# Attention with q and k laid out head dimension first, the output steps last in each tile's slot and the third part of the tiles in two banks

## The reference

```python
q_pool = q.reshape(B, H, S // 2, 2, D).mean(axis=3)          # B 2, H 8, S 1152, D 64
scores = scale * np.matmul(q_pool, k.transpose(0, 1, 3, 2))
attn = np.exp(scores - np.max(scores, axis=-1, keepdims=True))
attn = attn / (np.sum(attn, axis=-1, keepdims=True) + 1e-09)
attn_out = np.matmul(attn, v)                                # 16 heads of [576, 64]
x = attn_out.transpose(0, 2, 1, 3).reshape(B * S // 2, H * D)
x = (sigmoid(x @ w_gate) * (x @ w_val)) @ w_out              # 512 -> 1536 -> 512
# then 8 experts: out += P[:, e] * (relu(x @ w1[e]) @ w2[e]), P from a router
```

## Time and profile before

| | |
|---|---|
| median of 3 runs | 1294.13 us (1292.77 to 1295.09) |
| the profiled execution, its own time | 1293.19 us |
| its span in the profile | 1291.4 us |
| PE busy over the span | 1258.4 us (97%) |
| DVE, ACT, POOL busy over the span | 58%, 46%, 44% |
| attention: first exponential to last tile's exponential | 10.84 us to 292.33 us |
| granted TensorE clock in every slice | full |

### The profile page before, as it was taken

One profiled execution on the slowest core, in us unless ns is written; L12 is line 12 of the kernel. 1 busy time (PEld: TensorE's weight loads), 2 busy tenths in 40 slices (PEclk: granted clock), 3 DMA queues, 4 the chain that ended last, 5 costly groups with the idle time before them and its releaser, 6 DMA issues.

```text
span 1291.4 us, 20081 instructions
## 1 busy us (share of the span) xinstructions
PE 1258.4 (97%) x7716; PEld 1159.5 (90%) x7716; DVE 755.3 (58%) x1660; ACT 592.4 (46%) x1265; POOL 568.7 (44%) x336
## 2 busy tenths in 40 slices
PE   7999999989999999999999999999999999999999
PEld 6888888889999989999999899999998999999997
DVE  6888888885222313667656556556556465466443
ACT  6888888883333324444334334234333234234221
POOL 6466766680122247545325335335235245245211
PEclk9999999999999999999999999999999999999999
DMA  4334343211111043122222123123122122122112
GB/s 135 74 56 65 72 68 59 52 29 58 49 49 32 25 119 94 43 72 66 66 66 80 52 66 94 38 67 97 49 69 80 49 83 65 50 82 75 43 47 90
DMA packets 104090, 84.84 MB, mean 66 GB/s; under 512 B 14016, under 2 KB 80576, under 8 KB 104000
## 3 DMA queue, kind: packets, MB, share of 16 engines
q1 hardware_dynamic: 103856, 83.33, 24.3%
q10 hardware_dynamic: 144, 0.29, 0.1%
HBM read 79.15 MB, written 2.40 MB: 63 GB/s over the span
## 4 chain that ended last, share of the span: by engine, by line
PE 91%; DVE 4%; ACT 2%; issue 1%; POOL 1%; DMA 0%; SPq 0%; POOLq 0%; DVEq 0%; ACTq 0%
PE bank L957 11%; PE bank L959 11%; PE bank L958 11%; PE bank L1111 10%; PE bank L1112 10%; PE bank L1113 10%; PE bank L817 6%; PE bank L796 4%; PE bank L935 4%; PE bank L934 4%; PE bank L936 4%; PE bank L830 2%; PE bank L831 2%; PE bank L789 2%; DVE part_min L1441 2%
## 5 line engine op out<-in xcount | busy, mean ns | idle before, releaser
L1561 DVE TENSOR_TENSOR c<-bank,c 128x256 f32<-128x256 f32 (+1 forms) x448 | 197.2, 456 | 284.2 <-PE bank L959 273.7
L739 POOL TENSOR_TENSOR w_lo<-w_raw,w_hi 128x1024 fp32r<-128x1024 f32 x64 | 153.9, 2404 | 301.1 <-ACT w_hi L1128 301.1
L1112 PE MATMUL bank<-w_lo,h_hi 128*128 128x512 f32 x576 | 224.9, 390 | 0.0
L1111 PE MATMUL bank<-w_hi,h_hi 128*128 128x512 f32 x576 | 224.8, 390 | 0.0
L1113 PE MATMUL bank<-w_hi,h_lo 128*128 128x512 f32 x576 | 224.1, 389 | 0.0
L1299 ACT ACTIVATE h_hi<-c 128x256 fp32r<-128x256 f32 (+1 forms) x256 | 112.7, 445 | 165.9 <-DVE c L1561 165.6
L1113 PEld LDWEIGHTS bank<-w_hi,h_lo 128*128 128x128 f32 x576 | 108.2, 188 | 23.0
L1441 DVE TENSOR_REDUCE part_min<-bank 128x1 f32<-128x256 f32 (+2 forms) x216 | 109.0, 554 | 33.8 <-PE bank L831 32.2
L1111 PEld LDWEIGHTS bank<-w_hi,h_hi 128*128 128x128 f32 x576 | 108.2, 188 | 20.8
L1112 PEld LDWEIGHTS bank<-w_lo,h_hi 128*128 128x128 f32 x576 | 108.3, 188 | 20.1
L1128 ACT ACTIVATE c<-bank 128x256 f32<-128x256 f32 (+1 forms) x64 | 26.2, 409 | 209.9 <-PE bank L959 209.9
(11 more groups left out here) (154 smaller groups left out, 3100.5 us busy)
## 6 DMA issues: line engine op xcount, KB each, us to landing
w_raw<-in_moe_w SPq DMA_DIRECT2D x64, 512.0 KB, 3.6
w_raw<-in_moe_w SPq DMA_DIRECT2D x64, 256.0 KB, 3.1
wo_raw<-in_moe_w_out SPq DMA_DIRECT2D x16, 384.0 KB, 3.4
v_raw<-in_v SPq DMA_DIRECT2D x16, 288.0 KB, 3.2
k_raw<-in_k SPq DMA_DIRECT2D x14, 288.0 KB, 9.1
q_raw<-in_q SPq DMA_DIRECT2D x15, 256.0 KB
gv_raw<-in_moe_w_gate SPq DMA_DIRECT2D x12, 256.0 KB, 2.9
gv_raw<-in_moe_w_val SPq DMA_DIRECT2D x12, 256.0 KB, 3.2
```

The lines of the kernel that those rows point to most:

```text
L739: nc.gpsimd.tensor_tensor(w2_lo[:, u % 2], w2_raw[:], f32(w2_hi[:, u % 2]), ALU.subtract).then_inc(w2_split, 1)
L1111: nc.tensor.matmul(bank[:, 3 + i], hh, wh, start=first, stop=False)
L1112: nc.tensor.matmul(bank[:, 3 + i], hh, wl, start=False, stop=False)
L1561: nc.vector.tensor_tensor(dst[:, 0:w], bank[:, (u + b) % 3, 0:w], other[:, 0:w], ALU.add).then_inc(done, 1)
```

## The change

q and k are handed to the program in another layout, made on the host: for a head, q as [64, 2, 576] and k as [64, 1152], the head dimension first. Each is loaded twice, into partitions 0 to 63 and 64 to 127. The two planes of q are added to `q_sum` directly in the wanted layout. `fill_kq`, `kq_out` and POOL's K copy are gone: ACT writes the high part of K into a ring of three `k_st` straight from `k_raw` in two pieces (640 and 512 keys) and `q_hi` from `q_sum`; POOL (DVE for head 0) overwrites rows 0 to 63 of `k_st` with the low part; DVE forms `q_lo` in one piece of 576 from SBUF. The padding columns of `q_hi` and `q_lo` are zeroed once. PE's list of a tile becomes scores, the previous tile's three fills together, then nine output steps, in eight of the nine tiles; the third fill takes banks 5 and 6 in turn, so it waits for nothing. POOL's and SP's lists are written out for a pair of heads instead of one.

```diff
-AV_UPTO = (9, 18, 27, 36, 9, 18, 24, 30, 36)
+AV_STEPS = 9
+KPIECES = ((0, 640), (640, 1152))
+KRING = 3
...
+        def fill_bank(g, j):
+            if j < 2:
+                return 3 + j
+            return 5 + g % 2 if g < PAIR * NHEAD // 2 - 1 else 5
...
+            def load_q(h):
+                for half in range(2):
+                    sp.dma_start(q_raw[h % 2][rows_of(half)], q_dram[h]).then_inc(q_loaded[h % 2], 16)
+            def load_k(h):
+                for half in range(2):
+                    sp.dma_start(k_raw[h % 2][rows_of(half)], k_dram[h]).then_inc(k_loaded[h % 2], 16)
             def load_kq(h):
+                sp.wait_ge(q_summed[h > 2], max(h - 2, 1))
                 load_q(h)
-                sp.dma_start(k_raw[:], k_dram[h]).then_inc(k_loaded, 16)
+                sp.wait_ge(*k_there(h - 2, 2))
+                load_k(h)
...
+            def sum_q(h):
+                a = h % 2
+                pool.wait_ge(q_loaded[a], 32 * (h // 2) + 32)
+                if h >= 2:
+                    pool.wait_ge(q_lo_done, h - 1)
+                nc.gpsimd.tensor_tensor(q_sum[a][:], q_raw[a][:, 0], q_raw[a][:, 1], ALU.add).then_inc(q_summed[1], 1)
+            def split_k(h):
+                for piece in range(2):
+                    st, raw = k_of(h, piece)
+                    pool.wait_ge(k_hi_done, 2 * h + piece + 1)
+                    nc.gpsimd.tensor_tensor(st[rows_of(0)], raw[rows_of(0)], f32(st[rows_of(0)]),
+                                            ALU.subtract).then_inc(k_lo_done[1], 1)
+            def pair_of_heads(p):
+                h = 2 * p
+                split_k(h + 1)
+                split_v(h, 0)
+                if p >= 1:
+                    finish_head(h - 2)
+                if h < LAST:
+                    sum_q(h + 2)
...
+                split_v(h + 1, 1)
+                if p >= 1:
+                    pool.wait_ge(v_split, h + 2)
+                    finish_head(h - 1)
+                    pool.wait_ge(x_done, h)
+                if h < LAST:
+                    split_k(h + 2)
+                    sum_q(h + 3)
...
-                if i in (0, COMMON) and not first:
-                    pe.wait_ge(p_lo_done, 3 * g - 5)
-                    fill_p(prev, 0)
...
-                score(i, 2)
...
+                score(pair, i, 2)
+                if g >= 1:
+                    for j in range(NKB):
+                        if g >= 2 and j < 2:
+                            pe.wait_ge(p_lo_done, 3 * (g - 2) + j + 1)
+                        fill_p(g - 1, j)
+                if i < COMMON and pair >= 1:
+                    for n in range(AV_STEPS * i, AV_STEPS * (i + 1)):
                         av(h - 1, n)
...
+                if i > COMMON:
+                    for n in range(AV_STEPS * (i - COMMON - 1), AV_STEPS * (i - COMMON)):
+                        av(h - 1, n)
...
+            def between(pair, i):
+                h = 2 * pair
+                if i == 0:
+                    q_hi_part(h + 1)
+                if i in (1, 3) and pair >= 1:
+                    o_out(h - 1, 1, i // 2)
+                if i in (1, 2) and pair == 0:
+                    k_hi_part(1, i - 1)
+                if i == 6 or i == 8:
+                    o_out(h, 0, i // 2 - 3)
+                if h < LAST:
+                    if i == (3 if pair == 0 else 2):
+                        k_hi_part(h + 2, 0)
+                    if i == 4:
+                        k_hi_part(h + 2, 1)
+                    if i == 5:
+                        q_hi_part(h + 2)
+                    if i >= 7:
+                        k_hi_part(h + 3, i - 7)
+                elif i == 4:
+                    gv_hi_part(1, 0, 1)
...
+                if i in (1, 6) and h < NHEAD - 1:
+                    q_lo_part(h + 1)
```

More of the change, by code:

```diff
@@ L121, in pair @@
                 return allocate(s, [(f"{name}{a}", shape, dt) for a in range(2)])
-            q_sum = pair("q_sum", [PARTS, QT, 2, DIM], F32)
-            k_split = pair("k_split", [PARTS, KCH, 2, DIM], F32R)
-            k_st = pair("k_st", [PARTS, SEQ], F32R)
+            k_st1, q_raw0, q_raw1, v_raw, k_st0, k_st2 = allocate(s, [
+                ("k_st1", [PARTS, SEQ], F32R),
+                ("q_raw0", [PARTS, 2, QLEN], F32),
+                ("q_raw1", [PARTS, 2, QLEN], F32),
+                ("v_raw", [PARTS, KCH, DIM], F32),
+                ("k_st0", [PARTS, SEQ], F32R),
+                ("k_st2", [PARTS, SEQ], F32R)])
             q_hi = pair("q_hi", [PARTS, QT * PARTS], F32R)
@@ L207, in build @@
         w1_hi, w1_lo = (w1_hi0, w1_hi1, w1_hi2, w1_hi3), (w1_lo0, w1_lo1, w1_lo2, w1_lo3)
+        k_raw, q_raw, q_sum = (k_raw0, k_raw1), (q_raw0, q_raw1), (q_sum0, q_sum1)
+        k_st = (k_st0, k_st1, k_st2)
         gv_raw = [gv_raw0, gv_raw1]
@@ L367, in all_heads, with k_of, q_cols, k_there @@
                 head(h, h // 2, h % 2)
-        def pool_q(engine, a, src, done):
-            wide = [PARTS, QT, 2, DIM]
-            first = src[:, :, 0:DIM].unsqueeze(2).to_broadcast(wide)
-            second = src[:, :, DIM:2 * DIM].unsqueeze(2).to_broadcast(wide)
-            engine.tensor_tensor(q_sum[a][:], first, second, ALU.add).then_inc(done, 1)
-        def q_tiles(a):
-            return q_raw[:, 1 - a:QT + 1 - a]
+        def k_of(h, piece):
+            k0, k1 = KPIECES[piece]
+            return k_st[h % KRING][:, k0:k1], k_raw[h % 2][:, k0:k1]
+        def q_cols(a):
+            return slice(DIM * a, DIM * a + QLEN)
+        def k_there(h, pieces):
+            return k_lo_done[h > 0], 2 * (h - 1) + pieces if h else pieces
         def all_tiles(tile):
@@ L686, in gv_chunk0, with pair_of_heads @@
                 nc.gpsimd.tensor_tensor(chunk0[2], chunk0[0], f32(chunk0[1]), ALU.subtract).then_inc(gv_split, 1)
[L688 to L708 removed]
+            def pair_of_heads(p):
+                h = 2 * p
+                split_k(h + 1)
+                split_v(h, 0)
+                if p >= 1:
+                    finish_head(h - 2)
+                if h < LAST:
+                    sum_q(h + 2)
+                else:
+                    pool.wait_ge(q_lo_done, NHEAD)
+                    gv_chunk0()
+                split_v(h + 1, 1)
+                if p >= 1:
+                    pool.wait_ge(v_split, h + 2)
+                    finish_head(h - 1)
+                    pool.wait_ge(x_done, h)
+                if h < LAST:
+                    split_k(h + 2)
+                    sum_q(h + 3)
+            sum_q(1)
+            for p in range(NHEAD // 2):
+                pair_of_heads(p)
             gv_lo_part(1, 1)
@@ L820, in av, with score @@
                     mm.then_inc(av_done, 1)
-            def score(i, j):
+            def score(pair, i, j):
                 heads = (0, 1) if i == COMMON else (int(i > COMMON),)
@@ L876, in tile @@
-                f = i if i < COMMON else i - COMMON - 1
-                if f in (0, 2, 3):
-                    next_kq(h + 1, f)
-                if h >= 1:
-                    for n in range(0 if i in (0, COMMON) else AV_UPTO[i - 1], AV_UPTO[i]):
-                        av(h - 1, n)
-                if not first:
-                    if not second:
-                        pe.wait_ge(p_lo_done, 3 * g - 3)
-                    fill_p(prev, 2)
-                if f == 1:
-                    next_kq(h + 1, f)
@@ L1128, in copy, with q_hi_part, k_hi_part @@
                 return nc.scalar.activation(dst, src, ACT.Copy)
[L1132 to L1143 removed]
+            def q_hi_part(h):
+                act.wait_ge(q_summed[h > 0], max(h, 1))
+                nc.scalar.activation(q_hi[h % 2][:, q_cols(h % 2)], q_sum[h % 2][:], ACT.Copy,
+                                     scale=-SCALE).then_inc(q_hi_done, 1)
+            def k_hi_part(h, piece):
+                act.wait_ge(k_loaded[h % 2], 32 * (h // 2) + 32)
+                copy(*k_of(h, piece)).then_inc(k_hi_done, 1)
             def p_hi(g, j):
@@ L1200, in gv_hi_part @@
                 copy(gv_hi[a][:], gv_raw[a][:]).then_inc(gv_hi_done, 1)
-            act.dma_start(k_raw[:], k_dram[0]).then_inc(k_loaded, 16)
-            act.wait_ge(k_loaded, 16)
-            copy(k_split[0][:, :, 0], k_raw[:]).then_inc(k_hi_done[0], 1)
-            for f in range(FILLS):
-                kq_out(0, 0, f, 3 + f)
+            for half in range(2):
+                act.dma_start(k_raw[0][rows_of(half)], k_dram[0]).then_inc(k_loaded[0], 16)
+            k_hi_part(0, 0)
+            q_hi_part(0)
+            k_hi_part(0, 1)
             all_tiles(tile)
```

265 lines of the change are left out of this document (78 added, 187 removed).

## The result

| | before | changed kernel |
|---|---|---|
| median of the runs | 1294.04 us (1292.77 to 1295.09) | 1273.01 us (1271.52 to 1276.58, 4 runs) |
| ratio to before, 95% interval | | 0.9842 (0.982 to 0.9864) |
| the profiled execution, its span | 1291.4 us | 1271.5 us |
| first exponential, last tile's exponential | 10.84 us, 292.33 us | 14.35 us, 273.01 us |
| the 71 rounds between | 281.5 us | 258.7 us |

The kernel is 1.6% faster, 21 us by the medians, where 14 were forecast (1280, range 1269 to 1291). Behind the attention nothing changed: from the last tile's exponential to the end are 998.5 us, before 999.1.

A forecast was written before the change was run, and what follows sets the result against it. PE's necessary work a tile (3.23 us) and a round through three engines (3.31) were taken as nearly equal bounds. Rounds save 14.9, the start loses 1.0: 13.9 off the 1294.1 median gives 1280.2, range 1269 to 1291.

The forecast's parts named there:

- case (a): Whole kernel: time as forecast, with a `q_lo` wait between 0.5 and 1.1 us, 1276 to 1285; chance 0.50.
- Nine rounds at 3.31: Middle pair of heads: nine tile rounds through three engines at 3.31 us each, 29.8, with PE's 3.23 inside.
- Case (c): Attention rounds: three engines hold each other up in every round, 3.45 instead of 3.33, giving 1289 us; chance 0.23.
- The loose ends: Every round: small losses between three closely matched engines, 0.02 us each, 0.2 a pair.
- Tile 4: The tile holding both heads: six further score matmuls before its last minimum, 1.1 us more a pair.
- `q_lo`: DVE, twice a pair: 576 columns cost 0.68 less 0.20 to spare, 0.48 us each, 1.0 a pair.
- ACT's copies: ACT's `between`, 0.67 us free: 640 copies 0.09 each, tile 8's two copies 0.27, together 0.45 a pair.
- The wait w: DVE's `q_lo` stands still behind a POOL operation: 0.8 us each, bounds 0 and 1.43, 1.6 a pair.
- The rounds: All 71 attention rounds: 32.5 + 6 x 34.1 + 29.5 = 266.6 us, before 281.5, saving 14.9.
- The start: Up to the first exponential: 0.7 us shorter after landing, loads 1.7 later, net loss 1.0, bounds -1 to +2.3.
- (d): SP's queue: v lands late behind the store of reciprocals, making POOL late; slower, 1297 us and up; chance 0.08.
- case (b): DVE's `q_lo` finds POOL's port free, 13 x 0.8 = 10.4 us less, giving 1270; chance 0.15.

The follow-up runs named there:

- the kernel without gates: Changed kernel plus 64 dummy transposes at the start, start loads split over two queues and store of reciprocals on ACT; POOL doesn't wait for `q_lo`: 1274.42 us.
- its twin: Changed kernel plus 64 start transposes, two queues at the start, store on ACT, and `q_lo`'s first input from PSUM (right low part left out): 1264.19 us.
- the kernel of all four parts: Changed kernel plus 64 start transposes, two queues at the start, store of reciprocals on ACT, and POOL's waits for `q_lo`: 1264.35 us.
- `q_lo` from PSUM: Changed kernel with `q_lo`'s first input read from a PSUM bank instead of `q_sum`, leaving out the right low part of q: 1269.72 us.
- the kernel with layout and lists alone: Changed kernel with one bank for the third fill and that fill behind the output steps, as before the change: 1276.01 us.
- the two arrangements on queues: Changed kernel (SP loads q, ACT K at the start) against SP and ACT each loading one half of the partitions: 1273.01 and 1273.71 us.
- gates on POOL: Changed kernel with POOL waiting for `q_lo` before each head it finishes, next K split before the second finish: 1271.22 us.
- store alone: Changed kernel with the store of reciprocals issued by ACT in tiles 1 and 6 instead of by SP: 1271.73 us.

## Why the prediction was right, and where its sizes were off

The time is in the range and the likeliest case (a) has the right mechanisms, though the time itself, 1273, lies under its 1276 to 1285. The 7 us to the forecast are several mis-sized terms of both signs, and that a pair forecast too long and a start forecast too short partly cancel is luck. In the profiled execution the rounds are 7.9 shorter than forecast, the first exponential comes 2.5 later than forecast and the rest is 0.6 shorter: some 6 in all, from 1279.3 to 1273.4.

- **Nine rounds at 3.31**: 3.30 to 3.35, right in every tile without extras, though PE has no idle time in most of them. Case (c), 3.45, did not come. The loose ends, 0.2 a pair, are under 0.1.
- **Tile 4**, 1.1: its round is 4.34, 1.0 more.
- **`q_lo`**, 0.48 each: 0.33 (3.63 less 3.30). The operation takes 0.75, as forecast (0.76), but more of it is hidden than the 0.20 I read from one tile.
- **ACT's copies**, 0.45 a pair: 0.06, all of it in tile 8's round (3.36). I charged each copy with what exceeded 0.67 of free time, as if the fills' copies behind it had to start on time; they have slack.
- With these a pair without a held `q_lo` is 31.53, forecast 32.5.
- **The wait w**, 0.8: mechanism and place right, 0.45 in the mean of this execution, 0.55 to 0.79 in the kernel without gates beside its twin. "Slightly over the half" took POOL's operations as back to back; POOL waits for transfers in between. The bounds 0 and 1.43 held: the most was 1.2.
- **The rounds**: 258.7 against 266.6. Pairs 1 to 6 took 194.1 (48.48 to 242.56) where 204.6 were forecast; 5.8 of it are the pair of 31.53 in place of 32.5, 5.0 the smaller w (0.3 go the other way, mostly the round with ACT's wait for K). Pair 0 took 34.1, 1.6 more than forecast, for its two rounds at half rate (2.8). The last took 30.4, 0.9 more: PE's wait in the last round, which is 1.2 longer than a plain one, was in no term.
- **The start**, 1.0 lost: this step failed. It lost 3.5 up to the first exponential and 2.8 in the next two rounds, 6.3, above the bound of 2.3. Some 2.5 are the later landing (q's sum at 7.58 against 5.12, where I took 1.7). About 3.8 are PE's half rate: 2 x 1.41, and 1.0 between first scores and first exponential (11.10 to 14.35, 3.25; in the kernel of all four parts 2.25, before 2.24). The 0.7 that the new start was to save did not come: from q's sum to the first scores are 3.5 us before and after, since ACT takes K's first piece, which it gets at 8.80, ahead of `q_hi`. "No row shows a lower clock, and I count nothing" named the idle time and priced it at nothing. Before, the transposes of q and K had kept PE busy, so no row of that trace could show it.
- **(d)**: v lands after 8.8, as feared, and the slack was enough, though pairs are 2.6 shorter than forecast. Where no round was held up (`q_lo` from PSUM) its mechanism showed, by way of `o_other` rather than of v. Of case (b) half came true, seven of 13.
- What the removal of `fill_kq` and of the waits in front of output steps brings together is shown by the kernel with layout and lists alone, 18 us; no run takes the two apart. The order with its second bank is worth 1 to 3 us more, and without the bank costs 59.

The Trainium skill ("SBUF — State Buffer", Who interferes with whom) has a DVE instruction with two SBUF inputs contend with a GpSimd one that reads SBUF, and one with at most one SBUF input not. The pair of kernels with and without a PSUM input agrees, 747 against 1107 ns in the median. The Trainium skill ("SBUF — State Buffer", "Can I just issue two DMAs to hit both halves?") says that transfers to the two halves don't add their bandwidths. No run here loads one half alone; the loads at the start moved 226 and 238 GB/s in the two arrangements on queues, less than the 301 from 3 to 6 us before the change, which fits. The Trainium skill ("TensorE: Matmul & The Clock Gate", Wait — 56ns, not 53.3ns?) gives the spacing of matmuls as columns by 1.2 GHz for a cold array, which is 0.32 for 384; the trace has 0.32.

## What to carry to other kernels

Price an engine's idle time at the start by what the work behind it costs at TensorE's lower level, and look at the spacing of matmuls for it, since the granted clock's column can miss it; here 64 transposes of constants in place of 16 kept the first scores at the higher rate in all four kernels that had them. An operation of DVE with both inputs in SBUF should be given a place where POOL is known to wait for it: the gate cost POOL 24.5 us of waiting and the kernel nothing, and took 10 us off (1274.42 to 1264.35). With the store still in SP's queue the same gates brought 1.8 (1273.01 to 1271.22) with POOL's list late. While such a lock is free to fall, an improvement elsewhere of 3 us can't be read from the time; take the lock away first and then measure the rest.

## What was not expected of the hardware

- A granted clock given as 1.00 in stretches whose matmuls were spaced at half rate, from the first scores at 11.10 up to some time between 21.65 and 25.04, after PE had idled for 5.40. In the kernel with `q_lo` from PSUM the column has 0.50 from the first scores at 11.54 to 14.00. With 5.43 of idle time in another kernel the half rate lasted one round less.
- With 64 transposes at the start and its first scores at full rate, one execution (all but the gates, `q_lo` from PSUM) still fell to a granted clock of 0.50 from 16 to 18 us, and its first two rounds took 3.66 and 3.76. The three other kernels with the same transposes had the same wait of PE for the first exponential, 1.89, and none of it.
- DVE, held up by a POOL operation, went ahead of POOL's next one, which was then the longer: 1.93 in place of 1.42. Both engines lose by one meeting.
- With a store of 640 single numbers (2.5 KB) in SP's queue v's 288 KB landed after 8.8 and 10.2 us in the median (changed kernel, gates on POOL); with the store in ACT's queue after 5.8, 6.3 and 4.2 (store alone, all but the gates, the same with `q_lo` from PSUM).
